# Attention steps every 14 product steps instead of 12, a later third sum, and u sums moved over the tile border

## The reference, cut to what matters

```python
kv  = einsum('bhsd,bhse->bhde', k, v)           # 8 batches, 8 heads, 576 x 64
out = einsum('bhsd,bhde->bhse', q, kv)
a   = out / sqrt(mean(out*out, -1) + 1e-6) * g_norm
x   = a as (8, 576, 512)
h   = x.T @ U @ V                                # rank 32
u   = x + h.T
x2  = u + relu(u @ w_ch1) @ w_ch2                # 512 -> 2048 -> 512
h   = gelu(x2 @ w_in); u, v = halves of h
out = x2 + (u * (w_sg @ layernorm(v) + b_sg)) @ w_out
```

## Time and profile before

| | |
|---|---|
| median of 3 runs | 1368.72 us (1366.62 to 1369.74) |
| the profiled execution | 1368.81 us |
| its span, first to last instruction | 1367.0 us |
| mean granted TensorE clock | 0.992 |
| PE busy | 1307.4 us (96%) |
| DVE, ACT busy | 868.1 us (64%), 541.6 us (40%) |
| up stage | 45.8 us to about 559 us |

### The profile page before, as it was taken

The page is one execution under the profiler, slowest core; times in us unless marked ns, Lnnn a source line. Parts: engine busy times, 40 slices in busy tenths (PEclk is TensorE's granted clock), DMA queues, the critical chain, the costliest instruction groups (busy, mean ns, idle before and its releaser), DMA issues.

```text
span 1367.0 us, 22208 instructions
## 1 busy us (share of the span) xinstructions
PE 1307.4 (96%) x8590; PEld 1254.3 (92%) x8590; DVE 868.1 (64%) x1228; ACT 541.6 (40%) x892; POOL 97.9 (7%) x107
## 2 busy tenths in 40 slices
PE   5799999999999998999999999999999999999998
PEld 5688999999999988989999999998898998998987
DVE  4977575656565758888888888885642624425322
ACT  4554434444343432455444454535222322223221
POOL 6220000000000000000000000000210210111100
PEclk9999999999999999999999999999999999999999
DMA  9444445454545426736537174441012021120211
GB/s 233 126 139 130 148 132 155 131 165 149 163 131 158 131 96 217 274 124 221 173 104 257 55 271 146 162 154 60 19 60 79 10 77 39 49 77 23 66 39 39
DMA packets 182023, 170.27 MB, mean 125 GB/s; under 512 B 94112, under 2 KB 152496, under 8 KB 181952
## 3 DMA queue, kind: packets, MB, share of 16 engines
q1 hardware_dynamic: 178992, 164.42, 38.1%
q0 software_dynamic: 1600, 4.56, 1.2%
q10 hardware_dynamic: 1360, 0.30, 0.1%
HBM read 101.08 MB, written 66.06 MB: 122 GB/s over the span
## 4 chain that ended last, share of the span: by engine, by line
PE 83%; DVE 8%; ACT 3%; issue 2%; DMA 2%; SPq 1%; POOL 0%; DVEq 0%; ACTq 0%; POOLq 0%
PE ps L1366 24%; PE ps L1368 24%; PE ps L1367 24%; PE ps L1371 3%; PE ps L1395 2%; PE ps L1387 2%; PE ps L1403 1%; DVE w L1008 1%; DMA hT_scratch<-h_st 1%; DVE x_lo L1035 1%; DVE h_st L1059 1%; PE ps L1614 1%; PE ps L1615 1%; DVE y L975 1%; ACT w L702 1%
## 5 line engine op out<-in xcount | busy, mean ns | idle before, releaser
L1366 PE MATMUL ps<-x_hi,w 128*128 128x288 f32 x896 | 273.6, 305 | 26.4 <-DVE h_st L1059 7.5
L1367 PE MATMUL ps<-x_lo,w 128*128 128x288 f32 x896 | 266.3, 297 | 0.0
L1368 PE MATMUL ps<-x_hi,w 128*128 128x288 f32 x896 | 265.9, 297 | 0.0
L1366 PE MATMUL ps<-r_hi,w_hi 128*128 128x384 f32 x672 | 225.0, 335 | 3.0 <-DVE r_lo L1187 1.9
L1368 PE MATMUL ps<-r_hi,w_lo 128*128 128x384 f32 x672 | 224.5, 334 | 0.0
L1367 PE MATMUL ps<-r_lo,w_hi 128*128 128x384 f32 x672 | 224.5, 334 | 0.0
L827 ACT ACTIVATE r_hi<-hb 128x768 fp32r<-128x768 f32 x168 | 142.2, 848 | 169.3 <-PE ps L1368 164.3
L1366 PEld LDWEIGHTS ps<-x_hi,w 128*128 128x128 f32 x896 | 170.1, 190 | 31.8 <-DVE h_st L1061 7.9
L1367 PEld LDWEIGHTS ps<-x_lo,w 128*128 128x128 f32 x896 | 170.5, 190 | 0.0
L1368 PEld LDWEIGHTS ps<-x_hi,w 128*128 128x128 f32 x896 | 170.5, 190 | 0.0
L1329 DVE SCALAR_TENSOR_TENSOR vs<-ps,glcol,bias_bc 128x576 f32<-128x576 f32 x32 | 26.1, 815 | 199.8 <-PE ps L1615 199.5
(11 more groups left out here) (166 smaller groups left out, 2494.9 us busy)
## 6 DMA issues: line engine op xcount, KB each, us to landing
hT_scratch<-h_st SPq DMA_DIRECT2D x64, 576.0 KB, 4.7
hb<-hT_scratch SPq DMA_DIRECT2D x24, 1536.0 KB, 7.2
uT_scratch<-x_raw SPq DMA_DIRECT2D x32, 288.0 KB, 2.3
x_st<-uT_scratch SPq DMA_DIRECT2D x24, 384.0 KB, 3.5
x2T_scratch<-x_st SPq DMA_DIRECT2D x24, 384.0 KB, 6.8
x_raw<-x2T_scratch SPq DMA_DIRECT2D x8, 1152.0 KB, 6.0
k_raw<-in_k SPq DMA_DIRECT2D x64, 128.0 KB, 3.0
v_raw<-in_v SPq DMA_DIRECT2D x32, 256.0 KB, 3.0
```

The source lines that it names most:

```text
L1366: mm(dst, ws[0], xs[0], start=first, stop=False)
L1367: mm(dst, ws[0], xs[1], start=False, stop=False)
L1368: return mm(dst, ws[1], xs[0], start=False, stop=last)
```

## The change

`PERIOD` goes from 12 to 14 steps, one pair of heads for each group, and the places within it are QK 1, LOW 4, UT 7 and ATT 11 instead of 2, 8, 11 and (of the next period) 0. ACT copies q at 3 (was 2), behind the copy of product 1, takes `a_part`, q's tail and kv at 5, and after ATT at 11 the copies and squares. DVE has `sums`, `normalise`, `y_low`, `a_split` at 0, 1, 3, 6. The third sum of SBUF tiles (c22) follows the sum of product 5, so product 0 of the next group waits for sum 5 instead of 6. The u sums 6 and 4 and the low parts 2 and 3 go behind the border into steps 0 to 4 of the next tile, the low parts 4 to 6 from steps 0, 1, 4 to 5, 7, 8, and the high parts 4 to 6 to steps 5 to 7.

```diff
-PERIOD, QK, LOW, UT = 12, 2, 8, 11
+PERIOD, QK, LOW, UT, ATT = 2 * NI, 1, 4, 7, 11
 def hook(k):
-    r, at_ = divmod(k, PERIOD)
-    return (r, at_) if r < HP else (HP, -1)
+    return divmod(k, PERIOD)
...
 (ScalarE)
-            X_HIGH_AT = (HALF_UT + 2, HALF_UT + 4, LAST_UT + 4, LAST_UT + 5, LAST_UT + 8)
+            X_HIGH_AT = (23, 33, 53, 54)
+            X_HIGH_THEN = (5, 6, 7)
-                    if k < 2 and not first:
-                        x_high(t, par, 5 + k)
...
-                    if at_ == 0:
+                    if first and k == 0:
                         attn_copy(m, BX, BY)
                         squares(m, sq)
-                    elif at_ == QK:
+                    if at_ == QK:
                         std(m)
-                        if more:
-                            q_copy(m + 1, BX)
                     elif at_ == QK + 1:
                         y_high(m)
                     elif at_ == QK + 2 and more:
-                        act.wait_ge(s_kv, m + 2)
-                        q_copy_tail(m + 1, BY)
-                        kv_copy(m + 1, BY, P)
-                    elif at_ == LOW:
+                        q_copy(m + 1, BX)
+                    elif at_ == LOW + 1:
                         a_part(m, BX)
+                        if more:
+                            act.wait_ge(s_kv, m + 2)
+                            q_copy_tail(m + 1, BY)
+                            kv_copy(m + 1, BY, P)
                     elif at_ == UT:
                         u_evacuated(m, r, BX, 1 - par, t)
+                    elif at_ == ATT and more:
+                        attn_copy(m + 1, BX, BY)
+                        squares(m + 1, sq)
+                    if k in X_HIGH_THEN and not first:
+                        x_high(t, par, 4 + X_HIGH_THEN.index(k))
...
 (VectorE)
-                    dve.wait_ge(s_ad, NADD * n + 3)
-                    nc.vector.tensor_tensor(c22, c21, c22, ALU.add).then_inc(s_ad, 1)
                 elif idx == 5:
                     dve.wait_ge(s_ad, NADD * n + 4)
                     nc.vector.tensor_tensor(c12, p, c12, ALU.add).then_inc(s_ad, 1)
+                    nc.vector.tensor_tensor(c22, c21, c22, ALU.add).then_inc(s_ad, 1)
...
-            X_LOW_AT = (0, 1, 4)
+            def x_then(t, par, k, first=False):
+                if k == 0 and not first:
+                    x_sum(t, par, 6)
+                elif k in (1, 3) and not first:
+                    x_low(t, par, 2 + k // 2)
+                elif k == 4 and not first:
+                    x_sum(t, par, 4)
+                elif k in (5, 7, 8):
+                    x_low(t, par, 4 + (5, 7, 8).index(k))
...
-                    if at_ == 2:
+                    if at_ == 0:
                         sums(m, sq)
-                    elif at_ == 3:
+                    elif at_ == 1:
                         normalise(m)
-                    elif at_ == 4:
+                    elif at_ == 3:
                         y_low(m)
-                    elif at_ == LOW:
+                    elif at_ == LOW + 2:
                         a_split(m, BX)
...
+                    x_then(t, par, k, first)
+                    if k == 32:
                         x_sum(t + 1, 1 - par, 1)
+                    if k in (33, 54):
+                        x_low(t + 1, 1 - par, (33, 54).index(k))
+                    if k == 52:
                         x_sum(t + 1, 1 - par, 2)
...
 (TensorE)
-                if at_ == 0:
+                if first and k == 0:
                     pe.wait_ge(s_uev, m)
                     attention(m, BX, BY)
-                elif at_ == QK and more:
+                if at_ == QK and more:
...
+                elif at_ == ATT and more:
+                    pe.wait_ge(s_uev, m + 1)
+                    attention(m + 1, BX, BY)
...
-                        pe.wait_ge(s_ad, NADD * (n - 1) + (6, 7, 3)[idx])
+                        pe.wait_ge(s_ad, NADD * (n - 1) + (5, 7, 3)[idx])
```

More of the change, by code:

```diff
@@ L36 @@
 NX = NI + 2
-PERIOD, QK, LOW, UT = 12, 2, 8, 11
-LAST_UT = (HP - 1) * PERIOD + UT
-HALF_UT = PERIOD + UT
+PERIOD, QK, LOW, UT, ATT = 2 * NI, 1, 4, 7, 11
 TT = 768
@@ L843, in last_up_tile @@
                         copied(t, k)
-                    if k < 2:
-                        x_high(t, 1, 5 + k)
+                    if k in X_HIGH_THEN:
+                        x_high(t, 1, 4 + X_HIGH_THEN.index(k))
                     if k == 16:
@@ L1099, in up_tile @@
                         added(t, k)
-                    if k in X_LOW_AT:
-                        x_low(t, par, 4 + X_LOW_AT.index(k))
                     if first and g + 1 < NG and idx in (3, 6) and s_ == 0:
@@ L1105, in up_tile @@
                     m = HP * (t + 1) + r
-                    if at_ == 2:
+                    if at_ == 0:
                         sums(m, sq)
+                    elif at_ == 1:
+                        normalise(m)
                     elif at_ == 3:
-                        normalise(m)
-                    elif at_ == 4:
                         y_low(m)
-                    elif at_ == LOW:
+                    elif at_ == LOW + 2:
                         a_split(m, BX)
-                    if k == HALF_UT + 1:
+                    x_then(t, par, k, first)
+                    if k == 32:
                         x_sum(t + 1, 1 - par, 1)
-                    if k == HALF_UT + 9:
-                        x_low(t + 1, 1 - par, 0)
-                    if k == LAST_UT + 2:
+                    if k in (33, 54):
+                        x_low(t + 1, 1 - par, (33, 54).index(k))
+                    if k == 52:
                         x_sum(t + 1, 1 - par, 2)
[L1120 to L1127, removed]
             up_tile(0, 0, first=True)
@@ L1194, in last_up_tile @@
                         added(t, k)
-                    if k in X_LOW_AT:
-                        x_low(t, 1, 4 + X_LOW_AT.index(k))
+                    x_then(t, 1, k)
                     if k in (14, 15, 16, 18):
@@ L1441, in _, with attention_step @@
             u_transposed(3, 4, y_first[0])
-            def attention_step(k, t, end):
+            def attention_step(k, t, first, end):
                 r, at_ = hook(k)
@@ L1497, in up_tile @@
                     if not final:
-                        attention_step(k, t, end)
+                        attention_step(k, t, first, end)
             up_tile(0, 0, first=True)
```

## The result

The changed kernel takes 1390.32 us (median of 4 runs, 1388.69 to 1391.74), the kernel before 1368.75: a ratio of 1.0159, 95% interval 1.0146 to 1.0172. I had forecast the sign and a loss of 10 us; it lost 21.6 and lies above the range's end of 1387. The profiled executions differ by the same amount, 1389.0 against 1367.0 us of span.

What follows compares the result with a forecast made beforehand. TensorE's queue was taken to set the time. Removing 23.6 us and adding 30.4 in tiles 1 to 7 gave +6.8, tile 0 +3.3: 10.1 us on 1368.81, 1378.9 us, with an 8-in-10 range of 1366 to 1387.

Steps and rivals of the forecast that it cites:

- What goes: TensorE's waits for the sums of products 5 and 6 and the copy of u vanish: 23.6 us saved.
- LOW's wait for the copy of q: LOW waits as q's copy stands behind product 1's on ScalarE: 0.66 us a pair, 15.2 us in tiles 1 to 6.
- `y_low` decided only in tile 6's last pair: LOW waits for `y_low` only in tile 6's last pair, where there is no Q: 1.5 us.
- UT's wait for `a_split`: `a_split` stands behind product 2's sum on VectorE: 0.39 us a pair, 9.4 us; group 0's low part adds 4.0 us.
- The border: At tile borders, product 0's wait for the sum of product 5 goes: 9.8 us saved.
- Tile 0: First tile, its losses growing from 16.0 to 19.3 us: +3.3 us, with bounds of -3 and +8.
- the start: Start of tile 0: Q comes a step earlier but what it waits for does not; costs 3.8 us.
- UT's waits: In tile 0, weight splits and, in group 0, a low part stand ahead of `a_split`: 8.1 us.
- a rival with a chance of 0.12: Tile 0 takes more: delays chain on VectorE and the clock falls again, adding 5 to 8 us; chance 0.12.
- LOW's waits: In tile 0, LOW waits for the copy of q at 4 x 0.66 = 2.6 us.
- those for a weight half: In tile 0, product 0 waits for a group's second weight split, behind c22: 1.1 us at three groups, 3.3 us.
- Tile 7 and the rest: In tile 7, without attention, low part 4 is due at 6.4 us, ready at about 6.55: 0.25 us added.

Runs made afterwards that it cites:

- e1: Changed kernel with ScalarE's copy of q put back ahead of the copy of product 1: 1376.54 us, 1.0064 of before.
- e4: Changed kernel with the low parts at steps 5 and 33 moved one step later, behind `a_split`: 1378.98 us, 1.007 of before.
- e5: Changed kernel with copy of q and `a_split` put first, plus TensorE's loop over tiles 1 to 4 written out: 1350.55 us, 0.9869 of before.
- e8: Changed kernel with copy of q and `a_split` put first, plus tile 0's weight splits moved: 1344.36 us, 0.9827 of before.
- e9: Changed kernel, its queue order kept, with only tile 0's weight splits moved: 1380.25 us, 1.009 of before.
- e6: Kernel before with the third sum alone moved behind the sum of product 5: 1368.99 us, 1.0006 of before.
- e7: Kernel before, period of 12 kept, with third sum moved and x work spread over the border: 1378.79 us, 1.0077 of before.
- e10: Changed kernel with copy of q and `a_split` put first, but x work back in its old places: 1369.65 us, 1.0009 of before.

## Why the prediction was right in its mechanism and wrong in its size

The two new waits came where they were forecast, and the waits that were to go went. The time, 1390.3 us, lies above the 1387 that the range allowed, since terms of the sum were too small: tile 0's above all (3.3 us, measured 8.6), then UT's wait in group 2, the jump at the border and tile 7.

- **What goes** was right: the waits of the earlier trace rows and ATT's for the copy of u are gone in the changed kernel's tiles 1 to 6, and with nothing in their place a tile is 61.50 us.
- **LOW's wait for the copy of q**: forecast 0.66 a pair, measured 0.69, 27 times as said; undone by e1. The estimate by the Trainium skill, page "ScalarE: Activation LUTs", section "What ACT_TABLE_LOAD costs", 0.73, was no nearer. `y_low` decided only in tile 6's last pair, by 1.43 us and restart, forecast 1.5.
- **UT's wait for `a_split`**: forecast 0.39 and in group 0 1.06, measured 0.41 and 1.08. That they agree so well is luck in part: UT starts 0.14 us behind the end of `a_split`, not 0.05, and holds nothing back worth 0.10. **The term was mis-sized by one op**: I looked for low parts at step 5 of a tile, not at step 5 of each group, and missed the one at step 33. 0.67 in each of tiles 1 to 6, 4.0 us; e4 shows both.
- **The border**: "gone" was right for the wait and wrong for the time. Under one of the seven waits lay the loop's jump, of which the kernel before showed no more than a wait 0.4 longer than at the other borders. The sum took that wait off whole, and 1.9 us stayed; e5.
- **Tile 0** was the term that failed most: +3.3 forecast within -3 to +8, 8.6 measured. The tile is 10.6 us longer and begins 0.9 earlier, 9.7; 1.1 of that is an ATT that stood at the start of tile 1 before (each tile now holds the first ATT of the next, and tile 6 has one less). Against the forecast's list of losses, in its own terms:
  - the start costs 6.2, not 3.8. Q's data was there at 52.76 us, as before (52.85), though the tile began 0.9 earlier, and then the granted clock was 0.57 from 53 to 57 us.
  - UT's waits were 4.1, 3.3, 2.9 and 0.3, 10.6 in all, where I had 3.0, 2.35, 2.35 and 0.39, 8.1. In group 0 the weight split took 3.08 us, in group 1 2.31 and the cast in `a_split` 0.97 instead of 0.23, each while POOL made its sums; with POOL idle, in group 2, the split took the 2.02 of the earlier trace rows, and there the low part of step 33 was in the way. That POOL is what stretches them fits these rows, but no run has taken its sums away.
  - behind the first two of these waits the clock was at its lower level, 0.51 of full speed for 3.47 us and 0.50 for 2.93 us. Half of these stretches, an estimated 3.2 us, was lost. I had named that as a rival with a chance of 0.12 and left it out of the sum, which let 1.5 us stay for what the list did not explain.
  - LOW's waits (2.8, forecast 2.6) and those for a weight half (3.0, forecast 3.3) were right.

  Together 25.8 where I had 19.3; less the 0.9 of the earlier beginning that is the miss of 5.3 within 0.3. e8 and e9 show that most of UT's part hangs on the place of the weight splits.
- **Tile 7 and the rest**: -1.2 against -2.1, and tile 6 +1.7 with the moved ATT against +1.2.

The misses add: 4.0 for step 33, 1.9 for the loop, 5.3 for tile 0, 0.9 for tile 7, 12.1 in all, where 1389.0 - 1367.0 - 10.1 = 11.9 were to be found. All four have the same sign.

I had priced moving the third sum and the x work at nothing but what waits behind them. In the period of 14 that held but for the two low parts at step 5 of a group. In the period of 12 it would have misled: the third sum alone brings nothing (e6), with the x work it loses 10.6 us (e7), while with the places of the period of 14 the x work is worth 17.9 (e10). The loss of the change lies in two orders: undoing them gives back 38.6 us, more than the 21.6 that the change lost.

## What to carry to other kernels

Where one queue sets the time, read for every condition of that queue which op stands ahead of it in its own engine's queue, and when that op's own condition comes: an op that is ready but stands behind one that waits for the step before costs the length of both. List such ops by place in the period for every group of a loop body, not for the first alone. A wait that is to vanish may lie over something else, and the parts of a reordering can't be priced one at a time on the old order.

## What the runs showed of the hardware

A jump back at the end of TensorE's loop body of two tiles held up its products by 1.9 us, and not at all where the body was written out; in the kernel before, where TensorE waited there for VectorE anyway, the wait was only 0.4 us longer than at the other borders.

After a wait of 3.95 us the granted clock was 0.51 of full speed, the lower of its two levels (1.2 GHz of 2.4), from 0.8 us behind the wait's end for 3.47 us, with TensorE busy throughout; after one of 3.09 us it was 0.50 for 2.93 us. After another wait of 3.09 us, in e4, it was 1.00 (85.92 to 90.00 us), and after one of 2.72 us in the changed kernel too, so the length of a wait alone does not tell whether the clock falls. With waits of 0.2 to 1.7 us in the list it stayed at 1.00 over 337 us.

A subtraction of 128x1792 on VectorE took 3.08 and 2.31 us while POOL made sums, 2.02 us otherwise, and a cast of 128x128 0.97 instead of 0.23 us.
